# A read of solved blocks moved to another DMA queue, and the first pair's solve moved forward in the order of three engines

## What is computed

```python
for t in range(S):
    y[:, :, t] = np.einsum('bhd,bhde->bhe', rt, state)
    Sa = np.einsum('bhde,bhe->bhd', state, at)
    state_decay = state * wt[:, :, None, :] - np.einsum('bhd,bhe->bhde', Sa, bt)
    state = state_decay + np.einsum('bhd,bhe->bhde', vt, kt)
```

## Time and profile before

| | |
|---|---|
| three runs | 1060.81, 1055.99, 1068.70 us; median 1060.81 |
| profiled execution, its own time | 1065.29 us |
| span from first to last instruction | 1063.5 us |
| mean granted TensorE clock | 0.941 |
| PE busy | 924.9 us, 87% of the span |
| PE weight loads busy (they overlap) | 873.6 us, 82% |
| DVE, ACT, POOL busy | 631.1 (59%), 478.3 (45%), 217.9 us (20%) |
| DMA | 64.99 MB, mean 61 GB/s |
| read of dc | 12 issues of 256 KB on ACT's queue |

### The profile page before, as it was taken

One profiled execution on the slowest core, in us unless ns is written; L12 is line 12 of the kernel. 1 busy time (PEld: TensorE's weight loads), 2 busy tenths in 40 slices (PEclk: granted clock), 3 DMA queues, 4 the chain that ended last, 5 costly groups with the idle time before them and its releaser, 6 DMA issues.

```text
span 1063.5 us, 31728 instructions
## 1 busy us (share of the span) xinstructions
PE 924.9 (87%) x13408; PEld 873.6 (82%) x13408; DVE 631.1 (59%) x1087; ACT 478.3 (45%) x1011; POOL 217.9 (20%) x452
## 2 busy tenths in 40 slices
PE   3269696688688689788799999999999999999998
PEld 3268686687678589777789999999999999999998
DVE  8857555466456465365675665657566475655644
ACT  3246445435445455453563443535344353543533
POOL 8546623523523532400000000000000000000000
PEclk9688898898898899899899999999999999999999
DMA  5725462562473454223401000000000000000000
GB/s 154 153 41 130 103 140 69 100 148 69 103 161 92 105 123 95 49 91 97 140 14 26 1 26 26 1 25 0 25 0 25 25 0 25 0 25 5 9 14 13
DMA packets 143039, 64.99 MB, mean 61 GB/s; under 512 B 118940, under 2 KB 130076, under 8 KB 142924
## 3 DMA queue, kind: packets, MB, share of 16 engines
q1 hardware_dynamic: 93580, 60.16, 21.5%
q10 hardware_dynamic: 49344, 3.15, 3.3%
HBM read 45.98 MB, written 17.30 MB: 60 GB/s over the span
## 4 chain that ended last, share of the span: by engine, by line
PE 63%; DMA 15%; DVE 8%; ACT 6%; issue 5%; SPq 2%; POOL 0%; ACTq 0%; DVEq 0%; POOLq 0%
DMA dc<-d_scr 9%; PE acc L1116 5%; PE px L331 5%; DMA d_scr<-s_x 5%; PE acc L1117 5%; PE acc L1118 5%; PE mid L1116 3%; PE mid L1117 3%; PE mid L1118 3%; PE bank L1116 3%; PE bank L1117 3%; PE bank L1118 3%; PE pa L300 3%; PE pq L393 2%; PE pr L355 2%
## 5 line engine op out<-in xcount | busy, mean ns | idle before, releaser
L1469 DVE SCALAR_TENSOR_TENSOR stage<-mid,slopes 128x512 f32<-128x512 f32 x96 | 66.4, 691 | 107.1 <-ACT slopes L1310 107.1
L1306 ACT ACTIVATE stage<-mid 128x512 f32<-128x512 f32 x96 | 57.1, 595 | 160.2 <-PE mid L1187 160.2
L1116 PE MATMUL acc<-wo_h,act_h 128*128 128x320 f32 x384 | 121.5, 317 | 6.8 <-DVE act_l L1396 6.0
L1382 POOL TENSOR_TENSOR stats<-stats 128x1 f32<-128x1 f32 x24 | 13.2, 551 | 556.0 <-DVE stats L1444 556.0
L1117 PE MATMUL acc<-wo_h,act_l 128*128 128x320 f32 x384 | 118.5, 309 | 0.0
L1118 PE MATMUL acc<-wo_l,act_h 128*128 128x320 f32 x384 | 118.2, 308 | 0.0
L1116 PE MATMUL mid<-zT_h,w_h 128*128 128x256 f32 x384 | 108.6, 283 | 5.4 <-DVE zT_l L1396 5.4
L1117 PE MATMUL mid<-zT_h,w_l 128*128 128x256 f32 x384 | 108.2, 282 | 0.0
L1118 PE MATMUL mid<-zT_l,w_h 128*128 128x256 f32 x384 | 107.9, 281 | 0.0
L808 POOL TENSOR_TENSOR al<-al,prod 40x512 f32<-40x512 f32 x48 | 62.7, 1307 | 182.2 <-DMA al<-a_features_first 136.3
L1310 ACT ACTIVATE slopes<-stage,minus_alpha 128x256 f32<-128x256 f32 x192 | 87.4, 502 | 3.1
(11 more groups left out here) (163 smaller groups left out, 2475.0 us busy)
## 6 DMA issues: line engine op xcount, KB each, us to landing
wkb<-wkb_features_first SPq DMA_DIRECT2D x46, 242.5 KB
rvu<-rv_features_first SPq DMA_DIRECT2D x48, 160.0 KB
l_scr<-lb SPq DMA_DIRECT2D x24, 256.0 KB, 4.4
al<-a_features_first SPq DMA_DIRECT2D x48, 80.0 KB
sv<-v_time_first SPq DMA_DIRECT2D x48, 80.0 KB, 3.8
x_scr<-x SPq DMA_DIRECT2D x48, 80.0 KB
out<-y_sb SPq DMA_DIRECT2D x11, 320.0 KB, 2.3
d_scr<-s_x SPq DMA_DIRECT2D x12, 256.0 KB, 5.1
```

The costliest lines, as they stand in the source:

```text
L1116: pe.matmul(o, left[0], right[0], start=start, stop=False)
L1306: act.activation(neg[q % 2][:], mid[q % 2][:], ACT.Relu, scale=-1.0).then_inc(neg_ready, 1)
L1469: dve.scalar_tensor_tensor(out=act_f[q % 2][:], in0=mid[q % 2][:], scalar=0.0, in1=slope[q % 2][:], op0=ALU.max, op1=ALU.add).then_inc(act ...
```

## The change

Four things are changed. `d_read` moves from ACT's list to SP's: in steps 2 to 20 it stands behind l_read and ahead of load_wkb, in the prologue it follows its d_write directly. In odd steps d_write stands ahead of l_write. In the prologue l_read(0) stands ahead of load_a(4), and d_write(0) and d_read(0) ahead of l_write(1). DVE runs solve_first ahead of front(3), and front(4) is cut up and put between the stages of take_horner(0); PE runs all four horner stages and right_side(0) ahead of scores(4); ACT takes rhs(0) ahead of copy_l(4).

```diff
--- before.py
+++ after.py
@@ -222,6 +222,12 @@
             sp.dma_start(d_scr[p].rearrange("k l x -> l k x"),
                          s_x[:].rearrange("p k s t -> p k (s t)")).then_inc(d_out[p % 2], 16)
 
+        def d_read(p):
+            wait(sp, dd_ready, NB * p)
+            sp.wait_ge(d_out[p % 2], use(p, 2, 16))
+            blocks = d_scr[p].rearrange("k l x -> (k l) x").rearrange("(l b) (s t) -> (b s) l t", b=2 * NB, t=SB)
+            sp.dma_start(dc[:], blocks).then_inc(d_back[p % 2], 16)
+
         def save_y(m):
             sp.wait_ge(y_stored, m + 1)
             for h in range(2):
@@ -238,20 +244,22 @@
             load_a(3)
             load_wkb(3)
             l_write(0)
+            l_read(0)
             load_a(4)
-            l_read(0)
             load_wkb(4)
             for m in range(2):
                 load_v(m)
                 load_rv(m)
+            d_write(0)
+            d_read(0)
             l_write(1)
-            d_write(0)
             l_read(1)
             load_a(5)
             load_wkb(5)
             load_a(6)
             load_wkb(6)
             d_write(1)
+            d_read(1)
             load_wkb(7)
             l_write(2)
 
@@ -262,6 +270,8 @@
                 load_v(2)
             if n % 2 == 0 and n + 4 < NG:
                 l_read((n + 4) // 2)
+            if n % 2 == 0 and 0 < n < NG - 2:
+                d_read(n // 2 + 1)
             if n + 8 < NG:
                 load_wkb(n + 8)
             if n > 0:
@@ -275,10 +285,10 @@
         for n in range(NG):
             step(n)
             beside(sp, n)
+            if n % 2 == 1 and n + 3 < NG:
+                d_write((n + 3) // 2)
             if n % 2 == 1 and n + 5 < NG:
                 l_write((n + 5) // 2)
-            if n % 2 == 1 and n + 3 < NG:
-                d_write((n + 3) // 2)
         save_y(NG - 1)
 
     def tensor(pe, beside):
@@ -427,13 +437,11 @@
                 scores(m, 0)
                 scores(m, 1)
                 turn_kb(m)
-            horner(0, 0)
+            for stage in range(4):
+                horner(0, stage)
+            right_side(0)
             scores(AHEAD - 2, 0)
             scores(AHEAD - 2, 1)
-            horner(0, 1)
-            horner(0, 2)
-            horner(0, 3)
-            right_side(0)
             turn_kb(AHEAD - 2)
 
         def step(n):
@@ -600,18 +608,20 @@
             mask_both(0)
             front(2)
             mask_both(1)
+            solve_first()
             front(3)
-            solve_first()
             mask_both(2)
             mask_both(3)
-            front(4)
             take_horner(0, 0)
+            scan(4)
+            take_horner(0, 1)
+            invert_products(4)
+            take_horner(0, 2)
+            scale_kb(4)
+            take_horner(0, 3)
             scan(5)
-            take_horner(0, 1)
+            invert_products(5)
             mask_both(4)
-            take_horner(0, 2)
-            invert_products(5)
-            take_horner(0, 3)
             scale_kb(5)
             scan(6)
 
@@ -709,12 +719,6 @@
             for half in range(2):
                 act.copy(a_bd[ER[half], half], al[m % 7][ER[half], half]).then_inc(a_bd_ready, 1)
 
-        def d_read(p):
-            wait(act, dd_ready, NB * p)
-            act.wait_ge(d_out[p % 2], use(p, 2, 16))
-            blocks = d_scr[p].rearrange("k l x -> (k l) x").rearrange("(l b) (s t) -> (b s) l t", b=2 * NB, t=SB)
-            act.dma_start(dc[:], blocks).then_inc(d_back[p % 2], 16)
-
         def spread_d(p):
 
             act.wait_ge(d_back[p % 2], use(p, 2, 16))
@@ -752,21 +756,18 @@
                 if 0 < m < AHEAD - 3:
                     spread_a(m + 1)
                 take_kbn(m)
-            d_read(0)
             act.wait_ge(masks_loaded, 16)
             spread_d(0)
             spread_a(AHEAD - 2)
+            take_rhs(0)
             copy_l(AHEAD - 2, 0)
             copy_l(AHEAD - 2, 1)
-            take_rhs(0)
             take_kbn(AHEAD - 2)
 
         def step(n):
             front = n + AHEAD < NG
             take_u(n)
             take_uT(n)
-            if n % 2 == 0 and n + 2 < NG:
-                d_read(n // 2 + 1)
             if 0 < n and n + AHEAD - 1 < NG:
                 take_kbn(n + AHEAD - 1)
             if n == 0:
```

## The result

The changed kernel took 1017.1 us in the median of 4 runs (1014.0 to 1020.9), the kernel before 1061.8 us in 4 runs (1056.0 to 1068.7): a ratio of 0.9578 with a 95% interval of 0.9512 to 0.9645. The forecast was 1026, from 1005 to 1053. The span fell from 1063.5 to 1019.1, by 44.4 us.

What follows compares the result with a forecast made beforehand. The prediction took the dc read, slow beside the wkb load, and the stalls of ACT and PE behind it as the bound: 1065.3 - 30.7 (pairs 3 to 8) - 4 (pair 2) - 0 (front) = 1030.6, 1026 by the median; range 1005 to 1053.

Steps and rivals of the forecast that it cites:

- The read's time: Steps 2 to 14: the dc read on SP's queue ahead of the wkb load takes 5.55 us, as pair 9's.
- Rival A: In the steps, the dc read is not hastened and still takes 10 to 11 us; 1061 us, chance 0.12.
- The gain of a pair: Pairs 3 to 8, l_write to solve_u: mean 22.21 us falls to 17.10, six times 5.11, 30.7 us.
- Nor is the clock: Behind solve_u: no clock gain in the sum; after 2.51 us idle the clock is 0.50 for 3.8 us.
- Pairs 9 and 10: Late steps: their reads meet no wkb load, so they gain nothing.
- rival C: At solve_u: the stall goes almost wholly, read 4.5 us, clock no longer falls; 1002 us, chance 0.12.
- The front: Prologue: gives nothing, bounded by a gain of 3 us and a loss of 4; horner(0, 0) at 52.1.
- pair 2 +4: Pair 2: gains 6.0 us by the read, less 2 for l_write waiting for POOL's solve, so 4.
- solve(1) (14.0): POOL in the front: solve(1) takes 14.0 us, ending near 73.3, so scores(5) starts at 77.0.
- up to 4 if the solve comes 3 us later: Pair 2: what l_write pays for waiting behind POOL's solve; at least 0.8 us and the write's 0.4 issue.
- rival B: POOL's solve chain holds l_write(3) if horner(0, 0) starts at 57 or later; 1071 or 1036 us, chance 0.04.
- Covered: Front: s_in of pair 1 lands at 57 us, before POOL wants it at 59, so it costs nothing.

## Why the prediction was right, and where not

**The read's time** was the main step and it held: 5.55 was taken from the row of pair 9, 5.4 is the median. Two experiments bear it out from both sides, the read on SP behind the load (slower) and the read on ACT without the load (quick). Rival A is refuted. The row was one of two without a wkb load beside the read, though: in pair 10 the read took 7.00 before and 5.40 now, and with it l_write to solve_u went from 17.33 to 15.81, in a pair that was given no gain.

**The gain of a pair was mis-sized**: 5.11 was taken, 6.8 came in pairs 3 to 8. The sum took 17.10 from l_write to solve_u; measured were 16.73, 16.67, 15.57, 16.54, 16.98 and 15.40, mean 16.32, which makes 4.7 us over six pairs. The other 5.2 us lie in what I left as it was, from solve_u(3), (5), ... to the next l_write: 101.3 us in six stretches before, 96.1 after. Two of them, behind solve_u(9) and (13), took 14.03 instead of 17.10 and 16.71, and one, behind solve_u(11), 15.54 instead of 16.47; the other three were 1.5 us longer in all. The granted clock over 14 us from solve_u(5), (7), (9), (11) and (13) is 0.77, 0.78, 1.00, 0.88 and 1.00: the short stretches are the ones in which the clock stayed up. Timeline of PE, solve_u(5) and solve_u(9), and the 3.7 us behind each, in the columns of the earlier trace rows:

```profile
162.88 1.93 PE L365 MATMUL pr<-rhs,hh 64*64 64x40 f32 x32 [3.21 <-ACT rhs L685]
...
230.84 1.13 PE L365 MATMUL pr<-rhs,hh 64*64 64x40 f32 x32 [1.48 <-ACT rhs L685]
```

```profile
162.90:166.60 3.70, 3.70 (x65) 3.58 (x66) 3.60 (x6) 1.65 (x5) 3.46 (x4) 0.50 0.30 84
...
230.90:234.60 3.70, 3.70 (x86) 3.46 (x87) 3.60 (x6) 2.61 (x8) 3.54 (x3) 1.00 0.35 86
```

The term that was mis-sized is thus the gain of a pair, and the step that failed in it is "Nor is the clock": from "after the 2.51 of pair 9 it is 0.50 for the same 3.8 us" I left the clock out of the sum altogether. One row at 2.51 us of idle did not say what 1.5 does. Pairs 9 and 10 gave 4.7 us, forecast at nothing: 2.8 of them by the same, one stretch of 14.14 us behind solve_u(15) instead of 16.95, and 1.5 by pair 10's shorter read. So rival C was in part true: not its read of 4.5, but its clock, fully in three of the nine pairs, and for 2.7 to 3.1 us each time, not 1.7. In the kernel with the held loads the idle time is 0.9 to 2.6 in pairs 2 to 9, and solve_u takes 1.13 in pairs 3 to 9. That, with its front, is where its trace beats that of the change: its spans from l_write to solve_u (17.2, 16.0, 16.4 in pairs 3 to 5) are no shorter.

**The front** was given 0 with a loss of up to 4, and pair 2 +4; together -1.8 came. The chain as I had laid it out is there: horner(0, 0) at 51.0 (52.1 forecast) and scores(5) at 79.6 (77.0, and 76.42 before). The term that failed is "solve(1) (14.0)": it took 18.0, and solve(2) took 19.1 and ended at 112.5, 7.2 us later than before, where the text allowed "up to 4 if the solve comes 3 us later". Of the 7.2, 4.9 are a later start (l_write(2) stands at 84.1 instead of 79.2, behind the later scores(5)), and 2.3 its own length; the forecast gave that solve no length at all. l_write(3) stood behind d_write(2) and began at 112.94, 8.5 us later than before. In the chain:

```profile
112.48 0.40 SPq L222
112.94 0.64 SPq L206
113.62 4.39 DMA l_scr<-lb
118.08 0.39 SPq L214
118.56 6.04 DMA dc<-d_scr
```

So the mechanism of rival B worked in pair 2 alone, as it was bounded, and without the condition that I had given it (horner(0, 0) did not come late). "Covered" for s_in of pair 1 was wrong as well; it showed only once scan(4) was out of the way.

**Right besides:** no wait for the loads behind the read grew (DVE's scan 1.8 us for wkb, 1.5 before; POOL 87.7 for al, 136.3 before), pair 11 stalled nobody, and what lies behind solve_u(19) kept its time (632.95 and 632.1 us behind solve_u(19)). Part of the nearness is luck: a front forecast 5.8 us too good and pairs forecast 14.6 us too poor partly cancelled.

## What to carry to other kernels

When a small transfer stands on the critical path, look for an instance of it in the same trace that runs without the big one, and see what is issued beside it; either put the small one ahead in the same queue or hold the big one with a wait, which here did as much with the issuer left as it was. Then try the work that uses it behind what doesn't need it in its engine's list: moved one place too far back it was worth 1.2%, in its best place 2.7% on one kernel, and 0.2% on another. An operation moved forward pushes others back, and those must be followed through every engine; the last holder found is often one of two.

## What was not expected of the hardware

POOL's small instructions of the solve, 0.2 to 0.3 us each, now and then have a couple of slow ones, and there is more of that in the changed kernel, and as much in those with only the steps changed or only the loads held. Solve(2), timeline of POOL:

```profile
94.20 1.05 POOL L830 TENSOR_TENSOR s_t<-s_in,s_x 128x15 f32<-128x15 f32 x1
95.33 2.70 POOL L832 TENSOR_TENSOR s_x<-s_x,s_t 128x15 f32<-128x15 f32 x1
...
107.32 1.20 POOL L832 TENSOR_TENSOR s_x<-s_x,s_t 128x28 f32<-128x28 f32 x1
108.59 2.64 POOL L830 TENSOR_TENSOR s_t<-s_in,s_x 128x15 f32<-128x15 f32 x1
```

The solves of groups' pairs 3 to 9 have one such couple each (1.1 to 1.3 and 2.6 to 2.7 us), at other instructions each time; in the kernel before only one of these solves had it, and POOL stood idle 30.9 us in seven places ahead of scale_a without a cause that the profile shows. In the DMA records one packet of 16 KB on the instruction queue stands beside each of the two slow couples above (95.0 to 98 and 107.5 to 110.5). But one stands also at 119 to 122 in the kernel before, in the middle of a solve without a slow couple. That a fetch of instructions falls into the solve when POOL no longer stands idle beside it is only argued; no run tested it.

The length of the idle time does not by itself give the clock that follows: behind 2.60 us (solve_u(7)) solve_u took 1.93, behind 3.10 (solve_u(13)) 1.13, in the same execution. What else decides it is left open.
